# One w_out transpose moved in the head, and the last three tiles of the token phase regrouped and reordered

## The reference

```python
# attention, q, k, v: (4, 8, 576, 64); factor = 4
q_d, k_d, v_d = (mean over groups of 4 positions)
out_up = np.repeat(sm_attn(q_d, k_d, v_d), 4, axis=2)
mask = np.abs(pos[:, None] - pos[None, :]) < 4
attn_out = out_up + softmax(where(mask, scale * q @ k.T, -1e9)) @ v
x = attn_out.transpose(0, 2, 1, 3).reshape(2304, 512)
# first mixture: w_gate, w_val (512 x 1536), w_out (1536 x 512)
x = (1 / (1 + np.exp(-(x @ w_gate))) * (x @ w_val)) @ w_out
# second: phi (512 x 32), w1 (8, 512, 1024), w2 (8, 1024, 512)
logits = x @ phi
d = softmax(logits, axis 0)              # over the 2304 tokens
slot_input = (d.T @ x).reshape(8, 4, 512)
slot_out[e] = maximum(slot_input[e] @ w1[e], 0) @ w2[e]
out = softmax(logits, axis 1) @ slot_out.reshape(32, 512)
```

## Time and profile before

| | |
|---|---|
| median of three executions | 551.37 us (551.12 to 553.83) |
| profiled execution, its time | 553.79 us |
| its span on the core | 552.0 us |
| mean granted clock of TensorE | 0.985 |
| TensorE matmul busy | 528.6 us, 96% |
| VectorE, ScalarE, GpSimd busy | 225.4, 195.8, 106.8 us |
| bytes moved | 71.00 MB, 129 GB/s on average |

### The profile page before, as it was taken

The page is one execution under the profiler, slowest core; times in us unless marked ns, Lnnn a source line. Parts: engine busy times, 40 slices in busy tenths (PEclk is TensorE's granted clock), DMA queues, the critical chain, the costliest instruction groups (busy, mean ns, idle before and its releaser), DMA issues.

```text
span 552.0 us, 11786 instructions
## 1 busy us (share of the span) xinstructions
PE 528.6 (96%) x4770; PEld 404.1 (73%) x4770; DVE 225.4 (41%) x484; ACT 195.8 (35%) x530; POOL 106.8 (19%) x171
## 2 busy tenths in 40 slices
PE   5989999999999999999999999999999999999982
PEld 4768778877887787878777877878777788854431
DVE  0977965343643446253353527432223110140113
ACT  3757754242443243424233425233122212231022
POOL 8556253221212123112121212100000000000000
PEclk9979999999999999999999999999999999999997
DMA  9966963210311122011111110107006077599959
GB/s 207 231 159 153 341 131 89 67 44 14 77 47 45 45 45 67 23 47 44 47 44 45 45 47 0 27 1 287 18 0 213 17 262 275 215 397 394 400 192 342
DMA packets 86709, 71.00 MB, mean 129 GB/s; under 512 B 61312, under 2 KB 65920, under 8 KB 86656
## 3 DMA queue, kind: packets, MB, share of 16 engines
q1 hardware_dynamic: 86656, 70.25, 41.5%
HBM read 65.52 MB, written 4.72 MB: 127 GB/s over the span
## 4 chain that ended last, share of the span: by engine, by line
PE 85%; DMA 6%; SPq 2%; DVE 2%; issue 1%; ACT 1%; POOL 1%; DVEq 0%; ACTq 0%; POOLq 0%
PE gateb L1036 26%; PE valb L1036 26%; PE unitb L1046 4%; DMA ew_low<-in_moe_w_dram 3%; PE unitb L944 3%; PE unitb L989 3%; PE unitb L937 3%; PE unitb L1060 2%; PE unitb L1085 2%; DMA v<-in_v_dram 2%; PE unitb L973 2%; PE unitb L952 1%; PE unitb L1136 1%; PE unitb L979 1%; PE gateb L1154 1%
## 5 line engine op out<-in xcount | busy, mean ns | idle before, releaser
L1036 PE MATMUL valb<-w_hl,xhl 128*128 128x512 f32 x648 | 162.1, 399 | 0.0
L1036 PE MATMUL gateb<-w_hl,xhl 128*128 128x512 f32 x648 | 161.7, 398 | 0.0
L1036 PEld LDWEIGHTS gateb<-w_hl,xhl 128*128 128x128 f32 x648 | 118.3, 188 | 28.9 <-issue 4.1
L1036 PEld LDWEIGHTS valb<-w_hl,xhl 128*128 128x128 f32 x648 | 118.4, 188 | 25.0 <-issue 1.4
L851 DVE SCALAR_TENSOR_TENSOR hid<-hid,valb 128x512 f32<-128x512 f32 x54 | 37.1, 687 | 121.8 <-PE valb L1036 121.7
L730 ACT ACTIVATE hid<-gateb 128x512 f32<-128x512 f32 x54 | 32.2, 597 | 143.6 <-PE gateb L1036 143.6
L647 POOL TENSOR_TENSOR vd<-v 72x256 f32<-72x256 f32 x16 | 13.6, 850 | 103.6 <-PE unitb L973 87.5
L843 DVE TENSOR_TENSOR xhl<-xraw,xhl 128x512 fp32r<-128x512 f32 x18 | 12.8, 709 | 48.9 <-ACT xhl L658 48.8
L1046 PE MATMUL unitb<-ident,hid 128*128 128x128 f32 x216 | 31.9, 272 | 0.0
L658 ACT ACTIVATE hT<-unitb 128x512 f32<-128x512 f32 x54 | 31.7, 592 | 0.3 <-PE unitb L1046 0.3
L1046 PEld LDWEIGHTS unitb<-ident,hid 128*128 128x128 f32 x216 | 26.5, 140 | 6.8 <-issue 0.4
(11 more groups left out here) (179 smaller groups left out, 659.3 us busy)
## 6 DMA issues: line engine op xcount, KB each, us to landing
ew_low<-in_moe_w_dram SPq DMA_DIRECT2D x19, 1024.0 KB, 12.1
ew_high<-in_moe_w_dram SPq DMA_DIRECT2D x13, 1024.0 KB, 8.2
qtok<-in_q_dram SPq DMA_DIRECT2D x32, 144.0 KB, 2.7
ktok<-in_k_dram SPq DMA_DIRECT2D x32, 144.0 KB, 2.9
v<-in_v_dram SPq DMA_DIRECT2D x32, 144.0 KB
out_dram<-outs SPq DMA_DIRECT2D x18, 256.0 KB, 3.0
vloc<-in_v_dram SPq DMA_DIRECT2D x32, 112.0 KB
xraw<-in_moe_w_out_dram SPq DMA_DIRECT2D x12, 256.0 KB, 4.7
```

The lines of the kernel that those rows point to most:

```text
L1036: last = mm(bank[:, :], xhl[:, i % NX, x, kk, :], w_hl[:, c, m, w, kk, :], start=j == 0, stop=j == len(order) - 1)
```

## The change

In the head, `WT:2` is taken from its place before `S0:0` and put behind `Q1:1`, before `GP:1`.

In the last three tiles, chunk 0 stays as it was. The six gates of chunks 1 and 2 now all come before the six values. Each of the last four tiles is a group of its own. What ScalarE does for `LS` becomes a step `LX`, which stands right behind `LS` except for the last two groups. `alpha` has two columns, used in turn. Tile 16 uses the second place of `hT`. Of group 8 (tile 15) and group 10 (tile 17) the logits begin with chunks 0 and 1 (`LG0`). Three units (`TR` of tile 16's last chunk, `LS` of group 8, `LG` of group 9) are issued between the 12 matmuls of the last value. `keep_clock(8)` behind the last `LS` is gone, and `keep_clock(4)` comes behind the last two `SL` instead of the last. The places of the second chunk's value are filled behind those of the third chunk's gate.

```diff
-HEAD = """... WT:1 pool_Q:0 pool_K:0 WT:2 S0:0 Sd:0
-S1:0 mx0:0 mxd:0 k_in:1 exd:0 Q0:1 wo_in:3 Q1:1 GP:1 pool_V:0 ...
+HEAD = """... WT:1 pool_Q:0 pool_K:0 S0:0 Sd:0
+S1:0 mx0:0 mxd:0 k_in:1 exd:0 Q0:1 wo_in:3 Q1:1 WT:2 GP:1 pool_V:0 ...
...
-    for c in range(1, chunks):
-        ff += [("gate", (t0, c)), ("val", (t0, c)), ("gate", (t0 + 1, c)), ("gate", (t0 + 2, c)), ("val", (t0 + 1, c)),
-               ("val", (t0 + 2, c))]
+    ff += [(name, (i, c)) for name in ("gate", "val") for c in range(1, chunks) for i in range(t0, tiles)]
...
-    last_c, g = chunks - 1, len(groups) - 3
+    last_c, g = chunks - 1, len(groups) - 4
     n = place_of[("gate", (t0, 0))]
+    for at, *those in ((1, ("LG", g)), (2, ("LS", g), ("LX", g)), (3, ("ELT", g), ("TR", (t0, 0)), ("SL", g)), (6, ("TR", (t0 + 1, 0)))):
         put(n + at, *those)
     for c in range(1, last_c):
+        put(place_of[("val", (t0, c))] + 1, ("TR", (t0, c)))
+        put(place_of[("val", (t0 + 1, c))] + 1, ("TR", (t0 + 1, c)))
+    n = place_of[("val", (t0, last_c))]
+    put(n - 1, ("LG0", g + 1))
+    put(n, *[("TR", (t0 + 2, c)) for c in range(last_c)], ("TR", (t0, last_c)))
+    put(n + 1, ("LG", g + 1), ("TR", (t0 + 1, last_c)), ("LS", g + 1), ("LX", g + 1), ("LG", g + 2))
+    put(n + 2, ("LS", g + 2), ("ELT", g + 1), ("LG0", g + 3), ("TR", (t0 + 2, last_c)), ("SL", g + 1), ("LX", g + 2), ("LG", g + 3),
+        ("ELT", g + 2), ("LS", g + 3), ("SL", g + 2), ("LX", g + 3), ("ELT", g + 3), ("SL", g + 3))
...
+def inside_items(tiles, chunks, groups_n):
+    c, g = chunks - 1, groups_n - 3
+    last = ("val", (tiles - 1, c))
+    return {(last, 4): (("TR", (tiles - 2, c)), ("LS", g)), (last, 9): (("LG", g + 1),)}
...
+    GROUPS = [(i, GT) for i in range(0, TILES - 4, GT)] + [(i, 1) for i in range(TILES - 4, TILES)]
...
+        first_places = [*range(WO_SLOTS, W_PLACE + 6), VAL_HIGH - 2, VAL_HIGH - 1, W_PLACE + 6, W_PLACE + 7,
+                        X_PLACE + 1, VAL_LOW, VAL_HIGH, X_PLACE, *range(X_PLACE + 2, SLOTS)]
...
-            elif name == "LS":
+            elif name == "LX":
+                ub, free = banks[at["LS", arg][1]], bank_free[at["LS", arg][1]]
                 act.wait_ge(lmax_step, 3 * arg + 3)
                 if arg > 0:
                     wait_unit(act, ("ELT", arg - 1))
                     act.wait_ge(slot_sum, arg)
-                    wait_free(act, ("SL", arg - 1))
+                if arg > 1:
+                    wait_free(act, ("SL", arg - 2))
...
                     if j == lows - 1:
                         last.then_inc(low_used, 1)
+                    for between in inside.get((s, j + 1), ()):
+                        pe_step(pe, between)
...
-                if arg == GROUPS_T - 1:
-                    keep_clock(8)
...
-                if arg == GROUPS_T - 1:
+                if arg >= GROUPS_T - 2:
                     keep_clock(4)
```

More of the change, by code:

```diff
@@ L111, in program_steps @@
         if first + size < t0:
-            for at, name in ((2, "LG"), (3, "LS"), (5, "ELT"), (6, "SL")):
-                put(n + at, (name, g))
-    last_c, g = chunks - 1, len(groups) - 3
+            for at, *names in ((2, "LG"), (3, "LS", "LX"), (5, "ELT"), (6, "SL")):
+                put(n + at, *[(name, g) for name in names])
+    last_c, g = chunks - 1, len(groups) - 4
     n = place_of[("gate", (t0, 0))]
-    for at, *those in ((1, ("LG", g)), (2, ("LS", g)), (3, ("ELT", g), ("TR", (t0, 0)), ("SL", g)), (6, ("TR", (t0 + 2, 0)))):
+    for at, *those in ((1, ("LG", g)), (2, ("LS", g), ("LX", g)), (3, ("ELT", g), ("TR", (t0, 0)), ("SL", g)), (6, ("TR", (t0 + 1, 0)))):
         put(n + at, *those)
     for c in range(1, last_c):
[L120 to L127, removed]
+        put(place_of[("val", (t0, c))] + 1, ("TR", (t0, c)))
[6 more added lines that the diff above has]
+        ("ELT", g + 2), ("LS", g + 3), ("SL", g + 2), ("LX", g + 3), ("ELT", g + 3), ("SL", g + 3))
     def units(those):
@@ L252, in build @@
     GT = 2
-    GROUPS = [(i, GT) for i in range(0, TILES - 4, GT)] + [(TILES - 4, 1), (TILES - 3, 1), (TILES - 2, GT)]
+    GROUPS = [(i, GT) for i in range(0, TILES - 4, GT)] + [(i, 1) for i in range(TILES - 4, TILES)]
     GROUPS_T = len(GROUPS)
@@ L271, in build, with hT_place @@
     assert [arg for name, arg in body if name == "val"] == list(ff_n)
+    inside = inside_items(TILES, FC, GROUPS_T)
+    def hT_place(i):
+        return 1 if i == TILES - 2 else group_of[i][1]
     def hT_before(i):
-        g, t = group_of[i]
-        return max((n for n in range(g) if GROUPS[n][1] > t), default=None)
+        return max((group_of[n][0] for n in range(i) if group_of[n][0] < group_of[i][0] and hT_place(n) == hT_place(i)),
+                   default=None)
     ctx = ExitStack()
@@ L734, in act_step @@
                 wait_unit(act, s)
-                t = group_of[i][1]
-                if c == 0 and hT_before(i) is not None:
+                t = hT_place(i)
+                if i == TILES - 1 and c < FC - 1:
+                    act.wait_ge(lg_begun, 1)
+                elif c == (FC - 1 if i == TILES - 1 else 0) and hT_before(i) is not None:
                     wait_unit(act, ("LG", hT_before(i)))
@@ L1052, in pe_step @@
                 for r in range(FC):
-                    if arg == GROUPS_T - 1 and (r < FC - 1) != (name == "LG0"):
+                    if arg in (GROUPS_T - 1, GROUPS_T - 3) and (r < FC - 1) != (name == "LG0"):
                         continue
@@ L1059, in pe_step @@
                         f = CG * r + g
-                        last = mm(ub[g * NS:(g + 1) * NS, 0:size * P], gmat[:, f, :], hT[:, f, 0:size * P],
+                        last = mm(ub[g * NS:(g + 1) * NS, 0:size * P], gmat[:, f, :], hT[:, f, hT_place(first) * P:(hT_place(first) + size) * P],
                                   start=r == 0, stop=r == FC - 1)
+                if name == "LG0" and arg == GROUPS_T - 3:
+                    last.then_inc(lg_begun, 1)
                 if name == "LG":
@@ L1313, in _ @@
             for s in steps:
-                pe_step(pe, s)
+                if not any(s in those for those in inside.values()):
+                    pe_step(pe, s)
             pe_tail(pe)
```

14 lines of the change are left out of this document (7 added, 7 removed).

## The result

| | median | lowest to highest | executions |
|---|---|---|---|
| before | 550.31 us | 548.91 to 553.83 | 12 |
| changed | 553.05 us | 550.75 to 558.12 | 12 |

The ratio is 1.0052, with a 95% interval of 1.0028 to 1.0076: the change costs 2.7 us, half a per cent. As a difference it was +1.1 us against +2.7, and that is the gap to be explained. The higher starting value helped the level of the forecast by 1.06 us, which was luck. The profiled execution of the changed kernel took 551.89 us, 1.9 us *less* than the one of before (553.79). So one pair of profiles points the wrong way, and the first thing to read is why.

What follows compares the result with a forecast made beforehand. TensorE, busy 96% of the span, was taken as the bound. Head 0, last tiles +1.2, behind the last value +0.2 and tail -0.3 gave +1.1 us on 551.37: 552.5 us, range 549.8 to 554.8 us.

Steps and rivals of the forecast that it cites:

- all three signs that I had listed as wrong: S0:1 well before 17.8 us with earlier pooled scores; clock falling anywhere but 33 us; DMA idle time behind 485 us.
- Head, 0 (bounds -0.5 to +0.5): Head: moving WT:2 costs nothing, since the pooled scores at 33.74 us wait for GpSimd and v anyway.
- The new wait: Head, about 15 us: WT:2 waits for exponentials to read Sd:0's bank, a 0.8 us stop; S0:1 starts about 18.1 us.
- the figure 33.7: Head: the third pair's pooled scores would still come at 33.7 us.
- Up to the last value, +1.2: Last three tiles: LG of group 9 comes ahead (0.79 us) and two more restarts (+0.46 us); value ends at 485.6 us.
- hidden values that I had called ready in time: Last three tiles: 0.69 us on VectorE against 0.88 us of other transposes, so no transpose waits.
- Behind the last value, +0.2: Last value to last clock-keeping matmul: 10.0 us against 9.76, two passes round the engines replacing one.
- The stop: Behind the last value: TensorE stands 2.2 us before SL 8 for LS 9's bank, released by ScalarE.
- The tail, -0.3: Tail: TensorE comes 1.4 us later, weights still land at 533 us, so the last group's extra 0.32 us goes.
- DMA idle time behind 485 us: Tail weights: its appearance was listed as a sign that the forecast was wrong.
- rival (3): Clock falls in the stop at 15 us or 487 us: +3.2 us plus the tail's +1.1, 555.7 us; chance 0.12.

Runs made afterwards that it cites:

- e1: The kernel before with WT:2 moved in the head and nothing else: 550.20 us against 550.00, ratio 0.9995.
- e2: The changed kernel with the head of the kernel before: 552.89 us against 550.00, ratio 1.0057.
- e5: The changed kernel with six clock-keeping matmuls filling the stop before SL 8: 552.45 us against 549.62, ratio 1.0036.
- e10: The changed kernel with SL 8 in another bank, e3 unaltered in a later session: 552.99 us against 550.93, ratio 1.0026.
- e8: e3 with the three units inside the last value issued ahead of it instead: 551.99 us, ratio 1.0022.
- e9: The changed kernel, unaltered, run again beside the kernel before: 554.09 us against 550.93, ratio 1.0051.
- e4: The kernel before with seven unread products filling the stop before the third pair's pooled scores: 550.91 us against 550.00, ratio 1.0024.
- e3: The changed kernel with other banks set by hand for SL 8, the steps behind it and LS 10: 550.12 us against 550.00, ratio 1.0007.

## Why the prediction was right, step by step

The time was within the range, and would have been with the range put round 550.31 us as well (548.7 to 553.7). The difference was less than half of what came, and all three signs that I had listed as wrong appeared in some trace: early pooled scores, a clock that falls elsewhere, and DMA idle time. So the terms matter more than the sum.

**Head, 0 (bounds -0.5 to +0.5): right in the sum, wrong in its parts.** By e1's times the sum is +0.2 us. The new wait is there, with the releaser that I named, 0.93 us against the 0.8 foretold. But S0:1 came at 17.15 us, not at 18.1. The work from WT:2 to S0:1 took 2.5 us, against 2.6 foretold; it began at 14.66 us, 0.8 earlier than I had it. And the pooled scores came at 31.77 us, 2 us before their old place, which I had listed as a sign against me. e2 clears this up: with the old head they come at 31.75 us. What moved is GpSimd, which both kernels wait for. In the trace of before v landed at 27.64 us and the last two additions took 2.06 us. In the changed kernel's:

```profile
26.94 0.72 POOL L662 TENSOR_TENSOR vd<-v 72x256 f32<-72x256 f32 x1 [0.27 <-DMA v<-in_v_dram]
...
30.02 1.66 POOL L657 TENSOR_TENSOR qd<-qd,qT 128x144 f32<-128x144 f32 x2
```

Over all profiles the addition to `vd` starts between 26.75 and 27.90 us. The last two additions to `qd` take 2.06 us in before, e1, e5 and e10, and 1.65 to 1.67 in the eight others: both values occur with both heads. The four are the ones in which these additions began last, at 30.67 us or later, against 30.50 or earlier in the eight; what beside them makes the difference isn't shown. In e1 they are the late start and the long value, and the pooled scores come at 33.63 us. So this place is set outside TensorE, and the figure 33.7 was one draw of it; that it takes up TensorE's difference fits the times of e1 and isn't shown more closely.

**Up to the last value, +1.2: measured +1.56.** LG 9 ahead of the last value is 0.79 us, as its row was, and the two restarts 0.46. Two small terms were missing. The first two thirds and the last third of LG 8 (tile 15's group) are separate now, and the split costs 0.15 us (0.58 + 0.36 against 0.79). And the three transposes ahead of the last-but-one value (two of tile 17, then the last of tile 15) take 1.50 us, where three took 1.31:

```profile
472.06 1.50 PE unitb L1067 x12
...
476.32 0.36 PE unitb L1081 x8
```

The third waits for hidden values that I had called ready in time, by 0.88 us of cover against 0.69 us of VectorE's work: the cover was counted without the handing over. 0.79 + 0.46 + 0.15 + 0.19 = 1.59.

**Behind the last value, +0.2: measured +0.29.** The stop was put at 2.2 us and is 1.83, with the releaser that I named. The rest of the list took 8.2 us against the 7.8 foretold, spread over the hand-overs, so two misses of 0.4 us cancel.

**The tail, -0.3: measured -0.23.** The last group of L1175, the old L1154, in the chain:

```profile
528.87 2.02 PE gateb L1175 x16
```

It went from 2.22 us to 2.02 (1.98 in the timeline), not to 1.90. DMA idle time behind 485 us, which I had named as a sign against me, did appear, in a 2 us window of TensorE at 490 us with a DMA share of 0.75:

```profile
490.00:492.00 2.00, 2.00 (x19) 1.00 0.75 290
...
528.00:530.00 2.00, 1.72 (x18) 1.00 0.13 48
```

It was harmless here: by 528 us the share is 0.13, and no transfer stands in the chain of waits behind it. The stretch "to ysum" varies from profile to profile as well: it takes 39.5 to 39.9 us in ten of the twelve profiles and 40.1 in e8 and e10. The sign was badly chosen; it would have mattered only if the last transfer had come later.

**The sum.** The terms came to +1.6 us against +1.1 foretold. The medians say +2.7 and, again, +3.2 (e9). At least 1.1 us of that are in no term. The nearest thing that I had named is rival (3): I took its price, +3.2 us, from a fall in the head only, and gave the whole rival 0.12. What the traces show is a small fall. In three profiles of kernels with the bare 1.83 us stop (changed, e2, e9), two have a fall at 0.6 and 1.1 us behind it, each for +1.2 us on that stretch; in the nine others, where the stop is absent, shortened to 0.35 us or filled, there is none. The Trainium skill has a related case, in "TensorE: Matmul & The Clock Gate", Part 1, under "A second HAM failure mode: psum-queue depth-cycling": frequent short idle times between groups of matmuls, made by the turning round of banks in a bf16 kernel, make the clock go down and up again, at a cost. The traces of e2 and e9 agree in kind, with 1.83 us of idle time for a bank and 3.4 us at half clock behind it, though it is one stop here and not many; the changed kernel's trace has the same stop and no fall.

How the 2.7 us divide is settled in part. Read at equal mean clock, the changed kernel costs about what its terms say: a straight line through span against mean clock of the 93 executions of the kernel before (0.39 us of span for 1 us at half clock) has the twelve of the changed kernel 1.6 us above it on average, and e9's 1.9. The rest, 1.1 and 1.3 us by the medians, goes with a lower mean clock: 0.9887 and 0.9878 on average, against 0.9909 for the kernel before. These are estimates, and they don't say where the clock fell. The mean was as low in e1 (0.9888) and e10 (0.9888), which don't have the stop, and as high in e2 (0.9901), which has it, as in e4 (0.9902). A mean clock of 0.992 or more came in 11 of the 36 executions with the bare stop, in 49 of 96 of the other experiments, and in 58 of 93 of the kernel before, but in only 5 of 12 in e1. So it isn't shown that the stop *makes* the clock fall, nor that falls behind it are the missing 1 us; two of three traces against none of nine speak for it. e5, which fills the stop and was to decide it, shows no gain in the times.

e2 doesn't fit this account. It differs from the changed kernel only in its head, and lies 2.6 us above the same line. Four of its executions have a mean clock of 0.993 or more and a mean span of 550.85 us, 3.2 over those of the kernel before (547.67). A fall of 3.4 us, added to the 6.4 us or more at half clock that every profile has at its end, would put the mean at 0.991 (1 - 0.5 x 9.8 / 550); even on top of the highest mean on record, 0.995, it would leave 0.992. So by this estimate these four hold none. What costs them the 1.6 us beyond the terms stays open. What is shown: the terms are 1.6 us in the pair of profiles, a fall costs 1.2 us more where it comes, and the other bank takes 1.3 us out of its stretch in both traces.

**The regrouping itself.** e3 and e10 are the change with most of the stop gone: by e3's row +1.48 us up to the last value, -0.99 behind it (8.77 against 9.76) and -0.29 in the tail, together +0.2 us; by e10's, whose tail took 40.07 us, +0.8. Measured 1.0007 and 1.0026, and +0.4 us at high clock (548.05 against 547.67). Even so, the single groups give back behind the last value no more than they cost ahead of it. No kernel of this study is measurably faster than the one before.

## What to carry to other kernels

When steps are put into a new order by hand, follow the banks as well as the data: the stop before SL 8 was neither an operation nor a dependence, only a bank turned round four units later whose reader stood behind two other things on ScalarE, and other bank numbers took 1.3 us out of that stretch. Price a possible clock fall at each new stop by itself (1.2 us here, in two of three traces), and not by the one large fall that the trace of before happens to show. And before reading a head or a transfer as fixed, ask whether it is a draw: two profiles with the same head, of before and of e2, lay 5.3 us apart at H (88.61 and 83.33), twice what the whole change moves.

## What the runs showed of the hardware

- In 9 of the 12 profiles the granted clock fell in the head, first at some place between 31.3 and 45.9 us, with either head. I had expected one fixed place. 10.2 us at half clock went with 4.7 us at H (88.61 against 83.92), and 3.4 us in the tail with 1.2 us.
- e4's falling clock at 44.7 us came without any idle time over 1 us: 0.98 us before 41.79 and 0.58 us before 44.70 were the longest behind 18 us.
- The same two additions on GpSimd took 1.66 us in eight profiles and 2.06 in four, and the stretch with the 18 stores at the end varied by 1.7 us (17.97 to 19.66). Two profiles, one of each kernel, couldn't have shown a change of 2.7 us; twelve executions of the changed kernel, twice, gave 1.0052 and 1.0051.
